# Re-cutting and re-ordering the per-pair loads of a decay attention, and moving one vector product behind the scan in some pairs

## The reference

```python
# 1. decay attention, per (batch, head)
for t in range(S):
    cur = einsum('bhd,bhe->bhde', u * k_t, v_t)              # the bonus of the token itself
    y[:, :, t] = einsum('bhd,bhde->bhe', r_t, state + cur)
    state = w_t[..., None] * state + einsum('bhd,bhe->bhde', k_t, v_t)
x = y as (3072 tokens, 384)
# 2. soft mixture of 8 experts with 4 slots each (32 slots)
logits = x @ phi; slot_input = softmax over tokens(logits).T @ x
slot_out = relu(slot_input @ w1) @ w2, per expert
x = softmax over slots(logits) @ slot_out
# 3. gelu block: h = x @ w_in (384 x 2048); g = h * sigmoid(1.702 h); g @ w_out
```

## Time and profile before

| | us |
|---|---|
| median of 3 runs | 399.88 (398.59 to 404.15) |
| the profiled execution | 399.55 |
| its span on the core | 397.8 |
| the attention's pairs, start of the span to the last pair | about 0 to 134 |
| the experts | about 134 to 178 |
| the gelu block | about 178 to the end |

### The profile page before, as it was taken

The page is one execution under the profiler, slowest core; times in us unless marked ns, Lnnn a source line. Parts: engine busy times, 40 slices in busy tenths (PEclk is TensorE's granted clock), DMA queues, the critical chain, the costliest instruction groups (busy, mean ns, idle before and its releaser), DMA issues.

```text
span 397.8 us, 9113 instructions
## 1 busy us (share of the span) xinstructions
PE 387.3 (97%) x3482; PEld 309.7 (78%) x3482; DVE 242.9 (61%) x455; ACT 188.3 (47%) x422; POOL 49.0 (12%) x50
## 2 busy tenths in 40 slices
PE   6999999899999999999999999999999999999996
PEld 5877898898888643458888888888888888888885
DVE  4788887988887765257675554544545445454451
ACT  4877787887787423064444223322332242223321
POOL 3432342244224100000000000000000000000000
PEclk9999999999999999999999999999999999999999
DMA  7999999999998999930001000200020020002002
GB/s 274 380 375 375 385 391 360 316 402 361 309 397 344 371 415 407 415 139 1 2 0 50 31 0 2 80 1 0 0 79 0 0 79 0 2 0 79 2 1 79
DMA packets 15860, 68.68 MB, mean 173 GB/s; under 512 B 1744, under 2 KB 2896, under 8 KB 14800
## 3 DMA queue, kind: packets, MB, share of 16 engines
q1 hardware_dynamic: 15824, 68.18, 44.6%
HBM read 63.46 MB, written 4.72 MB: 171 GB/s over the span
## 4 chain that ended last, share of the span: by engine, by line
PE 87%; DMA 5%; DVE 4%; ACT 2%; issue 1%; SPq 0%; DVEq 0%; ACTq 0%
PE bank L1244 33%; PE bank L1248 16%; PE bank L1215 6%; PE bank L1023 5%; PE bank L1054 4%; PE bank L909 3%; DMA nat<-nat_in 3%; PE bank L1144 3%; PE bank L1164 3%; PE bank L1046 2%; PE bank L1005 2%; PE bank L990 2%; PE bank L930 2%; DMA rk<-rk_in 1%; PE bank L969 1%; PE bank L949 1%
## 5 line engine op out<-in xcount | busy, mean ns | idle before, releaser
L635 ACT ACTIVATE ring<-bank 128x512 f32<-128x512 f32 x96 | 57.4, 599 | 138.4 <-PE bank L1215 138.3
L876 DVE CAST g_split<-ring 128x512 fp32r<-128x512 f32 x96 | 41.0, 427 | 88.3 <-ACT ring L635 88.3
L1244 PE MATMUL bank<-g_split,wo_hi 128*128 128x512 f32 x285 | 80.1, 389 | 0.0
L1244 PE MATMUL bank<-g_split,wo_lo 128*128 128x512 f32 x285 | 80.0, 389 | 0.0
L1248 PE MATMUL bank<-g_split,wo_hi 128*128 128x512 f32 x285 | 80.0, 389 | 0.0
L878 DVE TENSOR_TENSOR g_split<-ring,g_split 128x512 fp32r<-128x512 f32 x96 | 66.4, 692 | 3.3
L1244 PEld LDWEIGHTS bank<-g_split,wo_lo 128*128 128x128 f32 x285 | 53.5, 188 | 11.1
L1248 PEld LDWEIGHTS bank<-g_split,wo_hi 128*128 128x128 f32 x285 | 53.5, 188 | 11.1
L1244 PEld LDWEIGHTS bank<-g_split,wo_hi 128*128 128x128 f32 x285 | 53.4, 188 | 11.2 <-DVE g_split L876 0.2
L1215 PE MATMUL bank<-cst,mst 128*128 (+1 forms) x96 | 37.4, 391 | 0.0
L447 POOL TENSOR_TENSOR nat<-nat 128x576 f32<-128x576 f32 x16 | 22.6, 1412 | 78.2 <-DMA nat<-nat_in 46.2
(11 more groups left out here) (164 smaller groups left out, 425.1 us busy)
## 6 DMA issues: line engine op xcount, KB each, us to landing
nat<-nat_in SPq DMA_DIRECT2D x32, 576.0 KB, 6.6
rk<-rk_in SPq DMA_DIRECT2D x16, 768.0 KB, 6.3
ring<-w_in SPq DMA_DIRECT2D x16, 768.0 KB, 7.6
w2a<-w_in SPq DMA_DIRECT2D x4, 1536.0 KB, 8.8
out_t<-ring SPq DMA_DIRECT2D x5, 768.0 KB, 3.5
ring<-w_in SPq DMA_DIRECT2D x6, 512.0 KB, 7.0
ring<-win_in SPq DMA_DIRECT2D x3, 1024.0 KB, 7.7
ring<-wout_in SPq DMA_DIRECT2D x4, 768.0 KB, 13.3
```

What stands on the lines that cost most here:

```text
L635: a.activation(gact[:, s % NG, :], bank[6 + s % 2][:, :], ACT.Gelu_apprx_sigmoid).then_inc(g_done, 1)
L876: v.tensor_copy(g_hi[:, s % NG, :], gact[:, s % NG, :]).then_inc(ghi_done, 1)
L1244: t.matmul(bank[3 * par + o][:, :], wo[:, f, P * o:P * (o + 1)], g_hi[:, s % NG, :], start=(f == 0 and wo is wo_hi), stop=False)
```

## The change

`nat` holds k, w, v, r in planes 0 to 3 instead of v, k, w, r (the host stacks them so; all users of the planes follow). The two transfers of 576 KB become three: `load_kw` (k and w, 576 KB), `load_v` (288 KB), `load_r` (288 KB). `load_kw` stands right behind `load_rk`, ahead of the weights, and waits for the first product of POOL of pair n-2 (`bonus_done`) and the logarithms that read its w (`ln_done`); `load_v` and `load_r` stand where `load_vk` and `load_wr` stood, with the waits those had. POOL and ACT wait for `ld_kw` instead of for the transfers that held k and w. `bonus` on DVE is split into `bonus_sums` and `bonus_values`; in pairs 3, 7 and 11 (`s.j == PPB - 1`) the second part is left out at the end of the pair and done in the next pair directly behind the scan, ahead of `x_out`.

```diff
@@ -152,8 +152,9 @@
 
         ld_rk = [sem(f"ld_rk{i}") for i in range(2)]
         ld_w = sem("ld_w")
-        ld_vk = [sem(f"ld_vk{i}") for i in range(2)]
-        ld_wr = [sem(f"ld_wr{i}") for i in range(2)]
+        ld_kw = [sem(f"ld_kw{i}") for i in range(2)]
+        ld_v = [sem(f"ld_v{i}") for i in range(2)]
+        ld_r = [sem(f"ld_r{i}") for i in range(2)]
         ld_u = sem("ld_u")
         ld_phi = sem("ld_phi")
         const_pool = sem("const_pool")
@@ -321,16 +322,22 @@
                     sp.wait_ge(inter_done, used)
                 sp.dma_start(rk[slot][:, :, :], rk_in[bass.ds(n, 1)].rearrange("a p q t -> (a p) q t")).then_inc(ld_rk[slot], 16)
 
-            def load_vk(n, slot, used=None):
+            def load_kw(n, slot, used=None):
+                if used is not None:
+                    sp.wait_ge(bonus_done, 2 * used - 1)
+                    sp.wait_ge(ln_done, used + 1)
+                sp.dma_start(nat[slot][:, 0:2, :], nat_in[bass.ds(n, 1), :, 0:2, :].rearrange("a p q n -> (a p) q n")).then_inc(ld_kw[slot], 16)
+
+            def load_v(n, slot, used=None):
                 if used is not None:
                     sp.wait_ge(y_done, 2 * used)
                     sp.wait_ge(av_done, used)
-                sp.dma_start(nat[slot][:, 0:2, :], nat_in[bass.ds(n, 1), :, 0:2, :].rearrange("a p q n -> (a p) q n")).then_inc(ld_vk[slot], 16)
-
-            def load_wr(n, slot, used=None):
+                sp.dma_start(nat[slot][:, 2:3, :], nat_in[bass.ds(n, 1), :, 2:3, :].rearrange("a p q n -> (a p) q n")).then_inc(ld_v[slot], 16)
+
+            def load_r(n, slot, used=None):
                 if used is not None:
                     sp.wait_ge(x_done, 2 * used)
-                sp.dma_start(nat[slot][:, 2:4, :], nat_in[bass.ds(n, 1), :, 2:4, :].rearrange("a p q n -> (a p) q n")).then_inc(ld_wr[slot], 16)
+                sp.dma_start(nat[slot][:, 3:4, :], nat_in[bass.ds(n, 1), :, 3:4, :].rearrange("a p q n -> (a p) q n")).then_inc(ld_r[slot], 16)
 
             def load_w1(m, q):
                 half = slice(q * (CM * FE // 2), (q + 1) * (CM * FE // 2))
@@ -344,21 +351,24 @@
             sp.dma_start(w0, w0_in).then_inc(ld_w, 16)
             load_rk(0, 0)
             sp.wait_ge(ld_w, 16)
-            load_vk(0, 0)
-            load_wr(0, 0)
+            load_v(0, 0)
+            load_kw(0, 0)
+            load_r(0, 0)
             sp.dma_start(ub[:, :, :], u_in).then_inc(ld_u, 16)
             load_rk(1, 1)
-            load_vk(1, 1)
-            load_wr(1, 1)
+            load_v(1, 1)
+            load_kw(1, 1)
+            load_r(1, 1)
             sp.dma_start(phi[:, :, :], phi_in).then_inc(ld_phi, 16)
             def two_pairs(m):
                 for q in range(2):
                     load_rk(2 * m + q, q, 2 * m + (q - 1))
+                    load_kw(2 * m + q, q, 2 * m + (q - 1))
                     load_w1(m, q)
                     if q == 1:
                         load_w2_early(m - 1)
-                    load_vk(2 * m + q, q, 2 * m + (q - 1))
-                    load_wr(2 * m + q, q, 2 * m + (q - 1))
+                    load_v(2 * m + q, q, 2 * m + (q - 1))
+                    load_r(2 * m + q, q, 2 * m + (q - 1))
 
             load_w1(0, 0)
             with sp.Fori(1, PAIRS // 2) as m:
@@ -438,9 +448,9 @@
 
                 if not s.first:
                     pool.wait_ge(av_done, s.i)
-                rb, kb = nat[s.slot][:, 3, :], nat[s.slot][:, 1, :]
-                pool.wait_ge(ld_vk[s.slot], 16 * s.loads + 16)
-                pool.wait_ge(ld_wr[s.slot], 16 * s.loads + 16)
+                rb, kb = nat[s.slot][:, 3, :], nat[s.slot][:, 0, :]
+                pool.wait_ge(ld_kw[s.slot], 16 * s.loads + 16)
+                pool.wait_ge(ld_r[s.slot], 16 * s.loads + 16)
                 if s.first:
                     pool.wait_ge(ld_u, 16)
                 pool.wait_ge(f_done, s.i + 1)
@@ -468,8 +478,8 @@
             def logs(s):
 
                 held = s.after(-1)
-                w = nat[held.slot][:, 2, :]
-                act.wait_ge(ld_wr[held.slot], 16 * held.loads + 16)
+                w = nat[held.slot][:, 1, :]
+                act.wait_ge(ld_kw[held.slot], 16 * held.loads + 16)
                 act.wait_ge(logsum_done, s.i)
                 a.activation(lw.rearrange("p c (h e) -> p (c h) e", h=HP)[:, :, 0:D],
                              w.rearrange("p (c e) -> p c e", e=D), ACT.Ln).then_inc(ln_done, 1)
@@ -721,6 +731,8 @@
                     dve.wait_ge(scaled, s.i)
                 v.tensor_tensor_scan(tsum[0:DP, :], frep[0:DP, :], bank[5][0:DP, 0:D * (NC - 1)], 0.0,
                                      ALU.mult, ALU.add).then_inc(state_done, 1)
+                if xg == 0:
+                    bonus_values(s.after(-1))
                 if not s.first:
                     x_out(s.after(-1))
                 for n, q in enumerate(MASKS):
@@ -728,7 +740,8 @@
                     v.tensor_tensor(at[:, 4 * q:4 * q + 4, :], bank[2 + q][:, :].rearrange("p (u t) -> p u t", u=4),
                                     causal[:, :].unsqueeze(1).to_broadcast([P, 4, P]), ALU.mult).then_inc(masked, 1)
                 if s.after(1) is None:
-                    bonus(s)
+                    bonus_sums(s)
+                    bonus_values(s)
                     running_max(b, bank[5])
                     logits_out(b, bank[5])
                     return
@@ -736,16 +749,22 @@
                 if xg == G3:
                     running_max(b, bank[4])
                     logits_out(b, bank[4])
-                bonus(s)
-
-            def bonus(s):
+                bonus_sums(s)
+                if s.j != PPB - 1:
+                    bonus_values(s)
+
+            def bonus_sums(s):
 
                 rb = nat[s.slot][:, 3, :].rearrange("p (u e) -> p u e", e=D)
                 dve.wait_ge(bonus_done, 2 * s.i + 2)
                 v.reduce_sum(asum[:, :], rb, AX.X).then_inc(asum_done, 1)
-                dve.wait_ge(ld_vk[s.slot], 16 * s.loads + 16)
+
+            def bonus_values(s):
+
+                rb = nat[s.slot][:, 3, :].rearrange("p (u e) -> p u e", e=D)
+                dve.wait_ge(ld_v[s.slot], 16 * s.loads + 16)
                 dve.wait_ge(asum_done, s.i + 1)
-                v.tensor_tensor(rb, nat[s.slot][:, 0, :].rearrange("p (u e) -> p u e", e=D),
+                v.tensor_tensor(rb, nat[s.slot][:, 2, :].rearrange("p (u e) -> p u e", e=D),
                                 asum[:, :].unsqueeze(2).to_broadcast([P, NC * HP, D]), ALU.mult).then_inc(av_done, 1)
 
             def x_out(s):
@@ -997,13 +1016,13 @@
                     y_transposes(s.after(-1))
                     pe.wait_ge(state_done, s.i)
                 n1 = s.after(1)
-                pe.wait_ge(ld_vk[s.slot], 16 * s.loads + 16)
+                pe.wait_ge(ld_v[s.slot], 16 * s.loads + 16)
                 for c in range(NC - 1):
                     if c in (0, 4):
                         pe.wait_ge(kcn_done, 2 * s.i + 1 + c // 4)
                     for h in range(HP):
                         ins = t.matmul(bank[5][HOFF * h:HOFF * h + D, 0:D * (NC - 1)].rearrange("p (e c) -> p e c", e=D)[:, :, c], kcn[:, c, HOFF * h:HOFF * h + D],
-                                       nat[s.slot][:, 0, HD * c + D * h:HD * c + D * (h + 1)], start=True, stop=True)
+                                       nat[s.slot][:, 2, HD * c + D * h:HD * c + D * (h + 1)], start=True, stop=True)
                 ins.then_inc(update_done, 1)
                 if n1 is None:
                     pe.wait_ge(xt_out, NC * b + NC)
@@ -1052,7 +1071,7 @@
                         for h in range(HP):
                             half = half_of(h, c)
                             ins = t.matmul(bank[6 + q][half:half + D, P * (c // 2):P * (c // 2 + 1)],
-                                           nat[s.slot][:, 0, HD * c + D * h:HD * c + D * (h + 1)], at[:, unit(h, CHUNKS.index(c)), :],
+                                           nat[s.slot][:, 2, HD * c + D * h:HD * c + D * (h + 1)], at[:, unit(h, CHUNKS.index(c)), :],
                                            start=False, stop=True, skip_group_check=True)
                     ins.then_inc(y_done, 1)
                 if xg == G3 and n1 is not None:
@@ -1285,7 +1304,7 @@
     arrays = {
         "rk_in": np.ascontiguousarray(np.stack([channels_first(r), channels_first(k)], axis=2)),
         "w0_in": tokens_first(w)[0],
-        "nat_in": np.ascontiguousarray(np.stack([tokens_first(v), tokens_first(k), np.roll(tokens_first(w), -1, axis=0), tokens_first(r)], axis=2)),
+        "nat_in": np.ascontiguousarray(np.stack([tokens_first(k), np.roll(tokens_first(w), -1, axis=0), tokens_first(v), tokens_first(r)], axis=2)),
         "u_in": np.ascontiguousarray(np.broadcast_to(u.reshape(1, H // 2, 2 * D), (P, H // 2, 2 * D))),
         "phi_in": rows_on_partitions(moe_phi),
         "w1_in": rows_on_partitions(moe_w1),
```

## The result

The changed kernel took 405.21 us in the median (403.80 to 411.39, 7 runs) against 399.88 (398.59 to 404.15, 7 runs): the ratio is 1.0133, with a 95% interval of 1.0100 to 1.0167. It is slower, by less than the 2% that count as clear. The forecast said 400.2 with a range to 403.0.

The account below looks back on a forecast made before the run. PE (7.36 us a pair) and the transfers (7.0 to 7.2) were taken as nearly tied. +0.7 +0.3 -0.3 -0.4 +0 = +0.3 us on 399.55 gave 399.85, as a median 400.2 us; range 397.3 to 403.0.

Parts of the forecast that it names:

- The order of bytes: Loads of a pair: w comes 1344 KB (3.4 us) sooner, v stands behind 288 KB more, 0.72 us later.
- This is not paid anew in each pair.: Updates waiting for v: they move 0.7 us later once, as the whole pair moves with it; +0.7 us.
- 0.3 of growth: Updates waiting for v: the shift grows if rk's issue moves too and the queue is empty by then; +0.3 us.
- rival B: Loop through rk holds every pair: 15.8 us for two pairs against 15.06, 4.8 us in all, 404.4 us; chance 12%.
- What I held against it: Objection to the loop through rk holding every pair: rk's 6.9 us landing holds queueing a starved loop would not have.
- What it gains: Line 909 finds the logarithms ready as w is in time: 0.26 us a pair at most, counted as -0.3 us.
- One more transfer: 0: Load queue, each pair: the extra transfer's first part and landing stay hidden while others are queued ahead; 0 us.
- The product behind the scan: -0.4: DVE behind pairs 7 and 11: scan 0.68 us sooner, line 1046's 0.48 us waits go; 0.4 of 0.96 us counted.
- ACT's wait for w gone: Profile sign at the logarithms: ACT's wait for `nat` gone, or nearly.
- Line 1005 waiting more than 1.6 us in total: Profile sign at the updates: PE's wait for a load longer than 1.6 us in total, up to 5.
- POOL's wait for its load: Profile sign on POOL: its wait for the load of k and r, 46.2 us before, not longer.
- The first gelu matmul: Profile sign: the first gelu matmul within 1.5 us of where it was.

Follow-up runs that it names:

- the order alone: The changed kernel with its moved product put back to the end of every pair, leaving only the new order of loads: 403.94 us, ratio 1.0092 to the kernel before.
- v-first order: Against the kernel before: three transfers, loads ordered rk, w1, w2, v, k with w, r, product at the end of every pair; 396.97 us, ratio 0.9906.
- the product alone: The kernel before with only the second part of `bonus` moved behind the scan in pairs 3, 7 and 11: 399.73 us, ratio 0.9999.
- v first: Here the run with loads ordered rk, w1, w2, v, k with w, r and the moved product, against the kernel before: 398.86 us, ratio 0.9964.

## Why the prediction was wrong, point by point

*The order of bytes.* Right, in kind and in the mean size: w is in time, and v stands 288 KB further back. I priced v at 0.72 us later. Over pairs 2 to 15 it landed 4.24 us behind rk before, in the mean, 4.98 in the change and 4.97 in the order alone: 0.74 later. Single pairs scatter far more. In pair 11 it was 93.6 - 89.8 = 3.8 us before (issued at 87.58 and 84.07, landing after 6.0 and 5.7 us) and 6.1 after, the most of any pair; bytes explain 1632 + 192 KB = 1.87 MB at 408 GB/s = 4.6 of these 6.1.

*"This is not paid anew in each pair."* This is the step that failed. I took the late v as one shift of 0.7 us with 0.3 of growth. The pairs are a loop: rk of pair n+2 is issued behind line 1046 of pair n, and that stands behind v of pair n. In the order alone the updates of pair 3 start at 35.05; rk of pair 5 is issued at 39.37 and lands after 5.5 us, and v lands at 51.05, 6.2 behind it. The updates of pair 5 start at 51.14, 16.1 us for two pairs that PE alone does in 2 x 7.36 = 14.7 at most. So the delay was paid again: waits for v of 5.5 us in that trace against 2.1 before, most of them in odd pairs, where w2 is ahead of v as well. The forecast had 1.0 us for all of it; the order alone lost 3.7 (1.0092) and the change 5.3. Three runs hold the cause from both sides: the same bytes ahead of v in another order are as slow (1.0108), v put ahead of k and w is faster than before (0.9906), and taking w2 out of the loop wins most of the loss back (1.0028).

This was rival B, at 12%, but only in part. It priced the loop at 404.4; the change measured 405.21 and the order alone 403.94. B wanted every pair held at about 7.9 us, and that is not what came: in the order alone pair 14 takes 130.78 - 123.42 = 7.36 us and pair 10 takes 98.50 - 91.10 = 7.40, unheld, beside 9.3 from the updates of pair 4 to those of pair 5 and 9.0 from 8 to 9. That its number is so near is luck in part. What I held against it, that 6.9 us of rk contains queueing, was right in the mean (6.0 us in the change, 6.2 before), though in pair 11 rk took 7.0.

*What it gains.* The 0.26 us a pair of earlier w were counted at 0.3 in all; no run isolates them. The v-first order moves v and w forward by 288 KB each, and gains 0.9% (0.9906) where the order of the change loses 0.9% (1.0092).

*One more transfer: 0.* Right (1.0002). The Trainium skill (DMA: Bandwidth & Descriptors, section Bandwidth) asks for transfers of 1 MiB or more, by figures for transfers that GpSimd issues (here SyncE does); no run here shows a cost of going from 576 to 288 KB behind a full queue.

*The product behind the scan: -0.4.* Wrong in both terms. The 0.48 us do go, twice, but I let the product sit ahead of `x_out` and the masks for nothing in pair 8 and wrote for pair 4 that the inter-state matmuls cover it. They don't: in the trace of the product alone PE waits 0.34 us for the masks in pairs 4 and 8 and 0.3 for the front behind pairs 4, 8 and 12, together 1.65 against the 1.0 that went. Part of it is `x_out` waiting for the product's own end (0.28 us in the timeline shown for v first), a wait that the old place hid behind the scan. The measured sum is 0 (0.9999), not -0.4.

*What was not in the sum at all: the clock.* I listed what the late v delays and took PE's rate as given. Behind an idle stretch of about 2 us in pair 2 the clock was at half. The Trainium skill (TensorE: Matmul & The Clock Gate, section Part 1, The HAM clock gate) says that an idle array falls to 1.2 GHz; the trace agrees in level. Its price can be smaller than it looks, since a slow PE also gives the loads time to get ahead: from 28 to 36 us the DMA share was 0.66, and the next updates did not wait. Keeping the clock up in pair 2 saved 1.1 us of 5.3 by the medians; the change's own runs at a mean clock of 0.987 took 1 to 3 us more than those at 0.992 to 0.996. How much of the 5.3 is the clock's stays open between these.

*The rest.* ACT's wait for w gone: as said. Line 1005 waiting more than 1.6 us in total: 5.7 (3.9 + 1.8), above the 5 I named. POOL's wait for its load is not longer (28.2 us against 46.2). The first gelu matmul, which was to stay within 1.5 us, came 11.9 later in the profiled execution (187.5 against 175.6). Pairs that nothing holds take 7.36 us as said. The product's effect on line 1046 as said, its return not.

## What to carry to other kernels

When loads and compute are nearly tied and each buffer is freed by the work that its predecessor fed, price a transfer by the bytes ahead of it in its queue, and run that through the whole loop from landing to the next issue; where the loop is longer than the engine's own time for it (here 16.1 us against 14.7), the delay is paid again. Run it with the spread from pair to pair, and not only with the mean. Put first what the bounding engine waits for, and split a transfer so that the late-needed half goes behind it, as v ahead of k and w did (0.9906), but see what the moved bytes then hold up: with v ahead of the weights too, the next rk came late and nothing was won (0.9993). Before moving a product out of one gap, look at what stands behind its new place, its own result's wait too.

## What the runs showed of the hardware

- Behind 2 us in which PE worked 0.62 us, waiting 1.75 us at a stretch for a load, its granted clock was 0.50 through the whole window from 28 to 36 us, while it was busy all the time. The waits of 0.8 us before left it at 1.00, and so did one of 1.83 us in the order alone (0.31 of 2 us worked) and one of 1.56 in the product alone.
- Three transfers of 288, 288 and 576 KB a pair ran as fast as two of 576 (1.0002, 0.9961 to 1.0044).
- Transfers of one queue overlap. In the stretch from rk's landing to v's in pair 11 of the change, 96.6 to 102.7 us, the queue moved more than stood ahead of v (packets, MB, share of 16 engines):

```profile
q1 hardware_dynamic: 736, 2.34, 99.6%
q8 instruction: 1, 0.02, 1.0%
```

  2.34 MB is 0.47 more than the 1.87 up to v, so bytes of transfers issued behind v (r and the next rk) went ahead of its last ones; at 408 GB/s that is 1.2 of the 1.5 us by which v came later than its bytes say. The one packet of another kind (1.0% of 16 engines in 6.1 us is 0.98 us on one engine) is not the reason for the difference: the same stretch before, 89.8 to 93.6 us, has one too, and there v came in 3.8 us with 1344 + 192 KB = 1.57 MB ahead of it, 3.9 us at 408 GB/s.
